# Gate and value products as seven block products per pair of tiles, with their weights split anew per chunk; last bias rows in steps of four

## The reference, cut to what matters

```python
scores = scale * q @ k.T                       # 4 batches, 8 heads, 576 x 576, head_dim 64
x = (log1p(|i - j|) / log1p(max(i, 1)))        # relative position
bias = relu(x * w1 + b1) @ w2                  # hidden 32 -> 8 heads, the same for all batches
attn = softmax(scores + bias) @ v
x = attn as [2304 tokens, 512]
gate = sigmoid(x @ w_gate); val = x @ w_val    # 512 -> 1536
out = (gate * val) @ w_out                     # 1536 -> 512
```

## Time and profile before

| | |
|---|---|
| time, median of 3 runs (lowest, highest) | 795.73 us (795.14, 796.69) |
| the profiled execution, its own time | 794.48 us |
| its span, first to last instruction | 792.6 us |
| mean granted TensorE clock | 0.998 of full |
| busy: PE, DVE, ACT, POOL | 770.5, 349.7, 345.3, 196.1 us |

### The profile page before, as it was taken

One profiled execution on the slowest core, in us unless ns is written; L12 is line 12 of the kernel. 1 busy time (PEld: TensorE's weight loads), 2 busy tenths in 40 slices (PEclk: granted clock), 3 DMA queues, 4 the chain that ended last, 5 costly groups with the idle time before them and its releaser, 6 DMA issues.

```text
span 792.6 us, 13855 instructions
## 1 busy us (share of the span) xinstructions
PE 770.5 (97%) x5308; PEld 641.4 (81%) x5308; DVE 349.7 (44%) x845; ACT 345.3 (44%) x684; POOL 196.1 (25%) x363
## 2 busy tenths in 40 slices
PE   7778999999999999999999999999999999999998
PEld 4336777777777777789889998998999899989996
DVE  7995777777777777625402220222022112302220
ACT  6996777667777677633312221222122112202210
POOL 0002666556545457768100000000000000000000
PEclk9999999999999999999999999999999999999999
DMA  5879333332432332224401001000200010000001
GB/s 137 197 187 200 78 100 83 80 95 64 123 75 71 78 82 59 66 82 121 132 28 54 1 1 55 25 1 14 67 1 0 17 64 1 1 26 14 1 1 40
DMA packets 86336, 49.92 MB, mean 63 GB/s; under 512 B 60160, under 2 KB 79744, under 8 KB 86272
## 3 DMA queue, kind: packets, MB, share of 16 engines
q1 hardware_dynamic: 85840, 48.96, 23.5%
q10 hardware_dynamic: 432, 0.09, 0.1%
HBM read 28.98 MB, written 9.44 MB: 48 GB/s over the span
## 4 chain that ended last, share of the span: by engine, by line
PE 85%; DMA 5%; DVE 3%; ACT 2%; POOL 2%; issue 1%; SPq 1%; ACTq 0%; POOLq 0%; DVEq 0%
PE f_ps L1080 19%; PE g_ps L1026 17%; PE u_ps L1026 16%; PE v_ps L1006 11%; PE so_ps L942 8%; PE ty_ps L955 4%; PE tx_ps L967 3%; DVE feats L726 3%; PE so_ps L937 2%; DMA bias<-bias_rows 2%; POOL w L527 2%; DMA x_raw<-in_w_out 1%; PE tx_ps L984 1%; PE v_ps L886 1%; PE ty_ps L896 1%; ACT feats L579 1%
## 5 line engine op out<-in xcount | busy, mean ns | idle before, releaser
L838 DVE TENSOR_TENSOR hid<-u_ps,sig 128x384 f32<-128x384 f32 x72 | 40.1, 557 | 243.4 <-PE u_ps L1026 243.4
L1026 PE MATMUL g_ps<-x_h,w 128*128 128x384 f32 x576 | 146.5, 335 | 0.0
L1026 PE MATMUL u_ps<-x_h,w 128*128 128x384 f32 x576 | 146.2, 334 | 0.0
L620 ACT ACTIVATE probs<-neg_scores,neg_max 128x576 f32<-128x576 f32 x144 | 111.1, 771 | 60.6 <-DVE neg_max L760 60.5
L510 POOL TENSOR_SCALAR probs<-probs,recip 128x512 f32<-128x512 f32 x128 | 88.6, 692 | 159.2 <-DVE recip L780 159.2
L1026 PEld LDWEIGHTS g_ps<-x_h,w 128*128 128x128 f32 x576 | 104.0, 188 | 0.8 <-POOL w L527 0.4
L1026 PEld LDWEIGHTS u_ps<-x_h,w 128*128 128x128 f32 x576 | 103.9, 188 | 0.5 <-issue 0.5
L688 ACT ACTIVATE h_h<-hid 128x384 fp32r<-128x384 f32 x72 | 37.9, 526 | 152.2 <-DVE hid L838 152.2
L1026 PE MATMUL g_ps<-x_l,w 128*128 128x384 f32 x288 | 96.3, 334 | 0.0
L1026 PE MATMUL u_ps<-x_l,w 128*128 128x384 f32 x288 | 96.2, 334 | 0.0
L760 DVE CUSTOM_DVE_ANT_0 neg_scores<-so_ps,bias 128x576 f32<-128x576 f32 x128 | 91.9, 755 | 5.4 <-PE so_ps L925 3.2
(11 more groups left out here) (92 smaller groups left out, 1147.5 us busy)
## 6 DMA issues: line engine op xcount, KB each, us to landing
bias<-bias_rows SPq DMA_DIRECT2D x12, 576.0 KB, 6.1
x_raw<-attn_transposed SPq DMA_DIRECT2D x6, 768.0 KB, 4.7
out<-out_sb SPq DMA_DIRECT2D x18, 256.0 KB, 2.0
q_raw<-in_q SPq DMA_DIRECT2D x32, 128.0 KB, 2.5
k_raw<-in_k SPq DMA_DIRECT2D x32, 128.0 KB, 2.5
v_main<-in_v SPq DMA_DIRECT2D x32, 128.0 KB, 2.3
w_raw<-in_w_gate SPq DMA_DIRECT2D x12, 256.0 KB, 3.0
w_raw<-in_w_val SPq DMA_DIRECT2D x12, 256.0 KB, 2.9
```

Source lines behind the costliest of these rows:

```text
L620: nc.scalar.activation(probs[s % RING][:, place, :], neg_scores[:, place, :], ACT.Exp, bias=neg_max[:, stat(s, place)], scale=-1.0, accum_ ...
L838: nc.vector.tensor_tensor(hid[f % 2][:, :], u_ps[f % 3][:, 0:CH], sig[f % 2][:, :], ALU.mult).then_inc(gated, 1)
L1026: last = nc.tensor.matmul(bank[f % 3][:, 0:CH], w[:, f, part, i, t, :], x[:, t, :], start=m == 0, stop=m == len(terms) - 1)
```

## The change

The third stage works on chunks of 768 tokens (3 chunks, each two blocks of 384), and on quads. A quad is one of the two products (gate for even n, value for odd n) for two feature tiles: a matrix of 2 x 2 blocks (tokens by features) with the inputs cut in two halves. In place of eight block products it takes seven (Strassen's scheme in Winograd's form): P1 to P7 multiply parts of x (A11, A12, A22 and the sums S1 to S4) by parts of the weights (B11, B21, B22 and the differences T1 to T4; A21 is used in the sums only). Each is 2 input slices by 3 terms, 6 matmuls of 384 columns. The partial results common to several blocks are kept: P1 stays in the PSUM bank Z, P6, P7 and P4 are added there, and ACT copies the bank to SBUF after P1, P6 and P7 (`keep_sum`), DVE adds P2, P3 or P5 from the banks X and Y (`sum_block`). A chunk has two phases of 6 quads, each followed by the outputs of its half of the features for 6 token tiles. The first half's outputs are kept in `out_sb` by ACT, the second half's added to them by DVE. In all there are 36 quads and 6 phases.

The weights are no longer kept. For each of the 36 quads SP loads 512 KB (`load_w`), POOL makes the differences T1 to T4 (`sum_w`, groups TA and TB) and the low parts of T (`low_w`), ACT the high parts (`high_w`), DVE the low parts of B. With x, the seven parts are made and split per chunk: by POOL in the attention for the first one, in the output phases by all three engines for the others. The output weights are split by ACT and DVE in quads 2 to 4 (first half) and by POOL in quad 6 (second half).

The last 64 bias rows are computed in steps of four rows rather than eight, with a table of logarithms of their own (`tail_win`, 583 KB more to load), so that each of their stores takes 16 rows at once, in 4 DMAs per duo.

The core of the diff:

```diff
+TAIL_STEP = 4
...
+CHUNK = 2 * CH
+CHUNKS = TOK // CHUNK
...
+PRODUCTS = {"P1": ("A11", "B11", "Z", True), "P2": ("A12", "B21", "X", True), "P6": ("S2", "T2", "Z", False),
+            "P5": ("S1", "T1", "Y", True), "P7": ("S3", "T3", "Z", False), "P4": ("A22", "T4", "Z", False),
+            "P3": ("S4", "B22", "Y", False)}
...
-TAIL_DMAS = 8
+TAIL_DMAS = 4
...
-                        for n in range(2):
-                            row = (1 - a) * REM + at + e + n * GRP
-                            sp.dma_start(bias_tail[row:row + 7 * ROW_STEP + 1:ROW_STEP, :, :],
-                                         bias_rows[i][n * P // 2 + a:(n + 1) * P // 2:2, e, :]) \
-                                .then_inc(bias_stored[i], 16)
...
+                        row = (1 - a) * REM + at + e
+                        sp.dma_start(bias_tail[row:row + (QU - 1) * TAIL_STEP + 1:TAIL_STEP, :, :],
+                                     bias_rows[i][a::2, e, :]).then_inc(bias_stored[i], 16)
...
+            def load_w(n):
+                at = n // 2 % PHQ * 2 * P
+                if n >= 2:
+                    sp.wait_ge(w_sums, 3 * (n - 1))
+                    for g in ("B1", "B22"):
+                        sp.wait_ge(w_ready[g], n - 1)
+                sp.dma_start(w_stage[:, n % 2, :, :], (wg, wv)[n % 2][:, at:at + 2 * P]
+                             .rearrange("(k p) n -> p k n", p=P)).then_inc(w_in[n % 2], 16)
...
+            for n in range(QUADS):
+                c = n // (2 * PHQ)
+                if n + 3 < QUADS:
+                    load_w(n + 3)
+                if n == 1:
...
+                    nc.gpsimd.tensor_tensor(t_raw[:, 0:2, :, :],
+                                            w_stage[:, n % 2, :, P:].rearrange("p (b k) n -> p b k n", k=KH),
+                                            w_stage[:, n % 2, 0:KH, :].rearrange("p k (b n) -> p b k n", n=P),
+                                            ALU.subtract).then_inc(w_sums, 1)
...
+                nc.gpsimd.tensor_tensor(t_raw[:, 1 + piece, :, :], of, less, ALU.subtract).then_inc(w_sums, 1)
...
+            def low_w(n, g):
+                pool.wait_ge(w_high[g], n + 1)
+                nc.gpsimd.tensor_tensor(w_part(n, 1, g), w_whole(n, g), plain(w_part(n, 0, g)),
+                                        ALU.subtract).then_inc(w_ready[g], 1)
...
+            for n in range(1, QUADS):
...
-                    split_w(u, piece)
+                    sum_w(n, piece)
+                for g in ("TA", "TB"):
+                    low_w(n, g)
+                if n == PHQ:
+                    for f in range(HFT, FT):
+                        split_wo(f)
+                if n % (2 * PHQ) == 0:
...
+            def high_w(n, g):
+                last = {"B1": "P2", "TA": "P7", "TB": "P4", "B22": "P3"}[g]
+                if g in ("TA", "TB"):
+                    act.wait_ge(w_sums, 3 * (n + 1))
+                else:
+                    act.wait_ge(w_in[n % 2], 16 * (n // 2 + 1))
+                if n >= 2:
+                    act.wait_ge(summed[last], n - 1)
+                nc.scalar.activation(w_part(n, 0, g), w_whole(n, g), ACT.Copy).then_inc(w_high[g], 1)
...
+            def keep_sum(n, product):
+                i, b = {"P1": (0, "11"), "P6": (1, "12"), "P7": (2, "22")}[product]
...
+                nc.scalar.activation(keep[:, i, :], z_ps[n % 2][:, 0:CH], ACT.Copy).then_inc(kept[product], 1)
...
+            for n in range(QUADS):
+                c, at = divmod(n, 2 * PHQ)
+                inside = n % PHQ > 0
+                more = 1 <= n < QUADS - 1
+                if inside:
+                    keep_sum(n - 1, "P7")
+                if more:
+                    high_w(n + 1, "B1")
+                if n:
+                    keep_sum(n, "P1")
+                if inside:
+                    block(n - 1, "22")
+                if more:
+                    high_w(n + 1, "TA")
+                if inside:
+                    block(n - 1, "21")
+                if more:
+                    high_w(n + 1, "TB")
+                block(n, "11")
+                if n:
+                    keep_sum(n, "P6")
+                if inside:
+                    block(n - 1, "12")
+                if more:
+                    high_w(n + 1, "B22")
+                if n in WO_QUADS:
...
+            def sum_block(n, b):
+                product, of, i = {"11": ("P2", "P1", 0), "22": ("P5", "P7", 2), "12": ("P3", "P6", 1)}[b]
+                bank = x_ps if b == "11" else y_ps
+                dve.wait_ge(summed[product], n + 1)
...
+                nc.vector.tensor_tensor(to, bank[n % 2][:, 0:CH], keep[:, i, :], ALU.add).then_inc(block_sum[b], 1)
...
+                nc.vector.tensor_tensor(block_tile(hid, b), of, block_tile(sig, b), ALU.mult).then_inc(hid_done[b], 1)
...
+            def low_h(n, b):
+                dve.wait_ge(h_high[b], n // 2 + 1)
+                nc.vector.tensor_tensor(h_block(h_l, n, b), block_tile(hid, b), plain(h_block(h_h, n, b)),
+                                        ALU.subtract).then_inc(h_ready[b], 1)
...
+            for n in range(QUADS):
+                c, at = divmod(n, 2 * PHQ)
+                inside = n % PHQ > 0
+                values = inside and n % 2 == 0
+                if n == 0:
...
+                    sum_block(n - 1, "22")
+                if values:
+                    hidden(n - 1, "22")
+                    hidden(n - 1, "21")
+                    low_h(n - 1, "22")
+                sum_block(n, "11")
+                if n % 2:
+                    hidden(n, "11")
+                if inside:
+                    sum_block(n - 1, "12")
+                if values:
+                    hidden(n - 1, "12")
+                    low_h(n - 1, "21")
+                if n % 2:
+                    low_h(n, "11")
+                if 1 <= n < QUADS - 1:
+                    low_w(n + 1, "B1")
+                if values:
+                    low_h(n - 1, "12")
+                if n < QUADS - 1:
+                    low_w(n + 1, "B22")
+                if n in WO_QUADS:
...
+            def product(n, name):
+                c = n // (2 * PHQ)
+                x, wp, bank, first = PRODUCTS[name]
...
+                    pe.wait_ge(block_sum["11"], n - 1)
+                if name == "P6":
+                    pe.wait_ge(kept["P1"], n + 1)
...
+                    if n >= 2:
+                        pe.wait_ge(block_sum["12"], n - 1)
+                if name == "P7":
+                    pe.wait_ge(kept["P6"], n + 1)
+                if name == "P4":
+                    pe.wait_ge(kept["P7"], n + 1)
+                if name == "P3":
+                    pe.wait_ge(block_sum["22"], n + 1)
+                    pe.wait_ge(w_ready["B22"], n + 1)
+                terms = [(t, wl, xl) for t in range(KH) for wl, xl in ((0, 0), (1, 0), (0, 1))]
+                for m, (t, wl, xl) in enumerate(terms):
+                    last = nc.tensor.matmul(quad_ps[bank][n % 2][:, 0:CH], wc[:, n % 2, wl, W_PARTS.index(wp), t, :],
+                                            xc[:, X_PARTS.index(x), xl, t, :],
+                                            start=first and m == 0,
+                                            stop=m == len(terms) - 1,
...
+                for name in EARLY.get(s, ()):
+                    product(0, name)
...
+            for n in range(QUADS):
+                ph = n // PHQ
+                inside = n % PHQ > 0
+                if n:
+                    product(n, "P1")
+                if inside:
+                    product(n - 1, "P4")
+                if n:
+                    product(n, "P2")
+                if inside:
+                    product(n - 1, "P3")
+                if n:
+                    for name in ("P6", "P5", "P7"):
+                        product(n, name)
+                if n % PHQ == PHQ - 1:
+                    if ph == 0:
+                        pe.wait_ge(x_ready[1], PAIRS)
+                    outputs(ph, 0, (0, 1, 2, 3))
+                    product(n, "P4")
+                    product(n, "P3")
+                    outputs(ph, 1, (0, 1, 2, 3))
+                    for i in range(2):
+                        outputs(ph, i, (4, 5))
+                    for i in range(2, OT):
+                        outputs(ph, i, tuple(range(HFT)))
 
```

More of the change, by code:

```diff
@@ L231, in program @@
         wo_h = sb("wo_h", [P, FT, DM], F32R, late)
+        with ExitStack() as whole_only:
+            wo_whole = sb("wo_whole", [P, FT, DM], F32, whole_only)
         wo_l = sb("wo_l", [P, FT, DM], F32R, late)
-        h_h = sb("h_h", [P, FT, CH], F32R, late)
-        h_l = sb("h_l", [P, FT, CH], F32R, late)
-        out_sb = sb("out_sb", [P, DM], F32, late)
-        hid = [sb(f"hid{i}", [P, CH], F32, late) for i in range(2)]
-        sig = [sb(f"sig{i}", [P, CH], F32, late) for i in range(2)]
@@ L241, in program @@
         late.close()
         with ExitStack() as banks:
[L243 to L252 removed]
```

(42 more changed lines are left out.)

582 lines of the change are left out of this document (357 added, 225 removed).

## The result

| | before | changed |
|---|---|---|
| median of 4 runs each (lowest, highest) | 795.43 us (794.28, 796.69) | 803.0 us (801.73, 805.94) |
| span of the profiled execution | 792.6 us | 800.8 us |
| mean granted clock in it | 0.998 | 0.996 |

The ratio is 1.010, with an interval at 95% of 1.0081 to 1.0119. The kernel became slower by 7.6 us, where 17.2 us less were forecast; the time lies outside the range of 757 to 797.

A forecast was written before the change was run, and what follows sets the result against it. PE was taken to bound the kernel. From 794.48 us, -37.4 - 1.2 - 2.2 + 0.5 + 6 + 13.5 + 3.6 = -17.2 gave 777.3, or 778.5 us as median; the 8-in-10 range was 757 to 797.

The forecast's parts named there:

- I take 0.45 us of stall per quad: Third stage's quads: DVE's low part of B reaches P1 late; 30 quads cost +13.5 us, bounds 0 to +57.
- Rival B: Quads: shared DVE/POOL path is the bound, POOL late, PE waits at P7, 1.1 us and more per quad, slower; chance 0.14.
- The rival's 34 us for the quads: Quads, by the skill page alone: shared path used 8.4 us per quad, 1.1 over PE, 30 quads cost 34 us.
- Matmuls, -37.4: Third stage's products: 1512 matmuls of 384 columns in place of 1728, 216 fewer at 0.1733 us, 37.4 us less.
- Transitions, +3.6: Each phase's end: PE waits for block 12 in `h_h` and `h_l`, +0.6 us for each of 6 (0 to +7).
- the w_out part: Ahead of the first outputs: the wait for loading, copying and splitting w_out's last part goes, -1.2 us (0 to -1.5).
- Start of the third stage, +6: First quads: ACT's late copy +2, quad 3's weights about 3 late, w_out split +1; together +6 us (1 to 12).
- the load order: First phase: quad 3's weights, queued behind 1.5 MB of w_out, land some 3 us later than ACT wants them.
- Chunk boundaries, put at nothing: Output phases: the parts of x for the next chunk are ready some 19 us into 26.6, so no cost.
- Bias stage, -2.2: Bias tail: 8 issues free SP earlier, DVE's wait at the third attention step goes, -2.2 us (0 to -3).
- Attention and filling, +0.5: Attention: POOL's split of x costs nothing (0 to +3); fewer products filling the last steps cost +0.5 us.
- Rival C: Quads: weights come too late by load latency, 0.5 to 0.8 us per quad on top, 785 to 795 us; chance 0.07.

The follow-up runs named there:

- e1: Changed kernel with POOL's differences and low parts written by memset from quad 1 on, reading nothing from SBUF, waits and signals kept: 763.96 us, ratio 0.960.
- e4: Changed kernel with DVE's low part of B moved ahead of block 11's sum and POOL's 512-element subtractions halved: 783.08 us, ratio 0.984.
- e2: Changed kernel with DVE's low part of B for the next quad moved ahead of the sum of block 11: 789.04 us, ratio 0.991.
- e3: Changed kernel with POOL's three subtractions of 512 elements per quad each cut into two of 256: 790.47 us, ratio 0.994.
- e10: Changed kernel with only the low part of TB moved from POOL to DVE: 800.29 us, ratio 1.006.
- e6: e4 plus the low part of TB moved from POOL to DVE, behind the sum of block 12: 773.47 us, ratio 0.971.
- e8: e6 with the load of quad 3's weights issued ahead of the first half of w_out: 770.79 us, ratio 0.968.
- e5: Kernel before with the bias part of the change alone: 794.12 us against 795.33, ratio 0.998.

## Why the prediction was wrong, step by step

**The step that failed: "I take 0.45 us of stall per quad".** The named place (the low part of B, P1 waiting) was right. So was the size of a wait: forecast 0.4, measured 0.39 us each. The step from these waits to PE's stop was not. By e1 against the changed kernel a quad that follows another lost (47.7 - 41.6)/5 = 1.2 us, 28.1 us in phases two to six and 9.3 in the first. The numbers for it stood in the prediction itself, for the even quads: the low part nominally ends at 6.4, P1 wants it at 7.28, four waits of 0.5 lie ahead, and 6.4 + 2.0 - 7.28 is 1.1 us. I then took less than half of it for all, as if collisions fell at random and the odd quads had none. In the traces both kinds have them, in phases two to five at the same places and with the same lengths within 0.02 us.

The first odd quad of the chain above is the simplest. P2 ends at 433.16 and the next P1 starts at 438.84. In these 5.68 us PE has four products of 1.04 us to do, 4.16. Behind P2 stands one chain: DVE's sum and product, ACT's copy, DVE's low part of h, DVE's low part of B. With e1's means it is 0.56 + 0.57 + 0.53 + 0.59 + 0.70 and some 0.2 of handoffs, 3.15 us, which leaves a slack of 1.0. The three waits in it add 1.13 + 0.38 + 1.0 = 2.5 us, and 1.5 of them reach PE. In the other odd quad the product of DVE misses POOL (0.57), the waits add 1.4, and 0.4 reach PE, as its stop of 0.42 shows. In the even quad DVE's product, low part and low part of B take 1.16, 1.64 and 1.21 us at one stretch (443.98 to 447.83), 2.2 more than undisturbed, and P1 starts at 447.89, again 1.5 late; with the slow start of 0.27 us behind the stop before it the quad is the 1.8 us longer that its 9.05 us show. The waits add up on one chain, and only the first microsecond of them is free. That they recur because the same product of PE releases ACT's copies for POOL and DVE's sum is what the orders suggest; no run here shifts one against the other and nothing else. The last phase shows how little it takes: with DVE first by 0.13 us, one of the stops is gone.

**Rival B** had the amount (1.1 us per quad and more, slower), with a chance of 0.14, but its mechanism, POOL late and PE stopped at P7, isn't the changed kernel's. There PE waited 4.3 us in all for ACT's copies. POOL's cycle became the bound only in e4, once the low part of B was off the chain and POOL's instructions were halved; e2 stops at P7 too, but because DVE's product is late, not POOL. That B's band (798 to 807) holds the measured 803.0 us is luck.

The Trainium skill (SBUF — State Buffer, Who interferes with whom) says that DVE and GpSimd share a port pair as an exclusive lock, and that whoever issues first gets it for the whole instruction while the other fully blocks. By that rule, the traces agree: DVE's 0.56 us became 1.68 and 0.97 beside POOL's subtractions of some 1.4 us, the rows at 453.86 and 754.52 show the loser change with the order of the starts, and e3 shows that a shorter instruction on POOL makes the wait shorter.

The rival's 34 us for the quads, worked out from that page, came close to the measured 37.4, but not for its reason. It added up the use of the shared path and compared it with PE's time per quad. e2 leaves that use as it is and gains 14 us, and e10 lowers it and gains 2.7, so it isn't the path's use that decided. For my own term I had put the row of 0.44 us in place of a full instruction, one collision beside a POOL instruction of 0.7 us, where the change has them of 1.3.

The other terms:

- **Matmuls, -37.4:** right. 240 matmuls take 41.6 us in e1, 0.1733 each. With the quads' term left out my sum was 763.8 us, as an own time; e1's profiled execution took 763.2. That closeness is in part luck: 3.6 us of transitions that didn't come made up for the bias stage's gain, which that execution doesn't show, and for about 2 us that I have no term for.
- **Transitions, +3.6: nothing.** All phases of e1 but the first show no wait ahead of the block 12 matmuls. In the first, one of 1.6 us is left (2.0 in the changed kernel), which eats the 1.2 us that the w_out part was to give back.
- **Start of the third stage, +6:** the first phase of e1 takes 67.7 us where PE's work alone is 63.0 (68.2 for 42 products and the outputs, less the five products done in the attention): 4.7, with the wait just named among them. Of it the load order, forecast at 3, was worth 2.7 with e6's orders (e8 against e6). Right in kind and size.
- **Chunk boundaries, put at nothing:** 1.1 us at each of two, in the changed kernel (outputs of a phase 28.15 us against 27.07 in e1). DVE's sums and low parts for the next x (mean 1.90 against 1.62 us) delay its additions to `out_sb`, for which PE waits 1.1 us. This is the same exclusion.
- **Bias stage, -2.2:** 1.2 by e5's medians, and its interval doesn't rule out 2.2. The wait of 2.2 us went, as forecast.
- **Attention and filling, +0.5:** the last values end at 347.6 us, before at 347.4. So the bias stage's gain doesn't show at the end of the attention of this execution. Some 0.8 us of it is the clock's dip in the bias stage (see e5). About 1 us goes between 272 and 289 us, where pieces of x and a difference of weights meet on POOL. That is read from the traces and wasn't tried.
- **Rival C:** no wait of PE ends with a DMA, and e1 and e6 run at full pace with the same loads from the second phase on. Late weights cost something once, quad 3's in the first phase: e6's chain of waits has a load of `w_stage` on it for 8.05 us from 349.08, and e8 moved it.

By measured terms the exclusion costs 9.3 + 28.1 + 2.2 = 39.6 us (the 9.3 with 1.6 us for a dip of the clock, last section), and e1, without it, is 31.5 us faster than before: the forecast of -17.2 fell between the two because it charged 13.5 for what cost 39.6.

## What to carry to other kernels

When a change puts POOL to work beside DVE, list DVE's instructions with two SBUF operands that lie between a matmul's end and the next matmul that needs their result. Add a full POOL instruction's wait to each and set the sum against the slack of that chain, not against busy shares. The cures that worked here, in this order of ease: take from the chain what needn't be in it (e2), shorten POOL's instructions (e3), and only then move work from POOL to DVE (e6 against e10).

## What the hardware did that I had not expected

The clock. In the first phase PE stopped for 1.37 us and then for 1.99 us, and after the second the granted clock fell, from about 387.8 to 391 us. The changed kernel, PE's timeline, then one stretch (columns as in the stretches above):

```profile
376.86 2.38 PE L1330 MATMUL z_ps<-xc,wc 128*128 128x384 f32 x12 [1.37 <-DVE wc L1017]
...
386.72 3.46 PE L1330 MATMUL z_ps<-xc,wc 128*128 128x384 f32 x12 [1.99 <-DVE wc L1017]
```

```profile
388.00:391.00 3.00, 3.00 (x11) 3.00 (x11) 2.21 (x4) 1.25 (x3) 0.26 (x1) 0.50 0.41 112
```

A clock of 0.50 is the lower of its two levels (1.2 of 2.4 GHz). The twelve matmuls behind the stop took 3.46 us on their row, against 2.38 behind the stop before. With the next six (1.70 against 1.20), the dip cost about 1.6 us, once. PE's stops of 1.5 us in the second phase left no such mark: the granted clock of that stretch is 1.00. Nor did a stop of 2.02 us ahead of 405.48, in the outputs of the first phase (clock 1.00 from 405 to 412), so the length of the last stop alone doesn't tell when the clock falls.

Such a dip isn't the changed kernel's alone, and it moves. The kernel before has one from 74.6 to 78 us, behind a stop of PE of 1.70 us; e5 and the changed kernel have one in the bias stage. So a difference of a microsecond between two profiled executions can be a dip that fell in one of them.
